# VectorE scales the values' sums one round later, and GpSimd's token operands move one round back

## The reference

```
scores = scale * q @ k.T + bias            # -1e9 outside the window
a = exp(scores - max);  a = a / (sum(a) + 1e-9)
x = a @ v                                  # then tokens x channels
h = x @ w_in;  g = h * sigmoid(h);         x = g @ w_out
h = x @ w_in2; g = h * clip(h + 3, 0, 6) / 6;  out = g @ w_out2
```

## Time and profile before

| | |
|---|---|
| median of 3 runs | 623.41 us (623.38 to 623.52) |
| the profiled execution's own time | 622.65 us |
| its span in the trace | 620.9 us |
| busy: PE, PEld, DVE, ACT, POOL | 94%, 84%, 59%, 54%, 43% |
| TensorE's granted clock | 1.00 of full speed |
| PE busy in the first seven fortieths of the span (0 to 108.7 us) | 80, 70, 70, 60, 70, 70, 60% |
| PE busy in the others | 90% or more, 80% in the last |
| attention on PE | from 5.6 us to about 121 us |

### The profile page before, as it was taken

One profiled execution on the slowest core, in us unless ns is written; L12 is line 12 of the kernel. 1 busy time (PEld: TensorE's weight loads), 2 busy tenths in 40 slices (PEclk: granted clock), 3 DMA queues, 4 the chain that ended last, 5 costly groups with the idle time before them and its releaser, 6 DMA issues.

```text
span 620.9 us, 9690 instructions
## 1 busy us (share of the span) xinstructions
PE 586.5 (94%) x3477; PEld 522.7 (84%) x3477; DVE 365.4 (59%) x680; ACT 335.8 (54%) x661; POOL 266.6 (43%) x279
## 2 busy tenths in 40 slices
PE   8776776999999999999999999999999999999998
PEld 5554555889999999999999998888888888888886
DVE  6455455787665566856755568557555685555431
ACT  5656556754444475644444657555555575445331
POOL 4344454565863333338633334377333333331110
PEclk9999999999999999999999999999999999999999
DMA  8333223013222212221221222222221242221002
GB/s 354 111 138 106 104 103 116 3 40 131 69 82 79 69 43 68 69 78 59 69 75 64 66 69 69 68 70 68 69 69 68 69 150 88 69 68 35 0 1 101
DMA packets 14596, 50.05 MB, mean 81 GB/s; under 512 B 1619, under 2 KB 1875, under 8 KB 14547
## 3 DMA queue, kind: packets, MB, share of 16 engines
q1 hardware_dynamic: 14258, 48.63, 23.1%
q10 hardware_dynamic: 288, 0.79, 0.4%
HBM read 46.27 MB, written 3.15 MB: 80 GB/s over the span
## 4 chain that ended last, share of the span: by engine, by line
PE 87%; ACT 4%; DVE 4%; issue 3%; DMA 1%; ACTq 0%; POOL 0%; DVEq 0%; SPq 0%
PE ps L1038 37%; PE ps L1125 22%; PE ps L1116 13%; PE ps L1117 7%; PE ps L1010 4%; PE ps L986 3%; ACT probs L763 2%; DVE negs L564 1%; ACT probsT L774 1%; PE ps L995 1%; DVE g_lo L694 1%; DMA k_raw<-in_kT 1%; DVE g_f L552 1%; PE ps L976 1%; DVE wi_lo L527 0%
## 5 line engine op out<-in xcount | busy, mean ns | idle before, releaser
L383 POOL TENSOR_TENSOR wo_lo<-wo_raw,wo_hi 128x1024 fp32r<-128x1024 f32 x32 | 77.1, 2410 | 262.4 <-ACT wo_hi L825 255.6
L1038 PE MATMUL ps<-x_hi,wi_hi 128*128 128x384 f32 x448 | 151.2, 337 | 0.7 <-DVE c_sb L542 0.3
L1038 PE MATMUL ps<-x_hi,wi_lo 128*128 128x384 f32 x448 | 150.0, 335 | 0.0
L1038 PE MATMUL ps<-x_lo,wi_hi 128*128 128x384 f32 x448 | 150.0, 335 | 0.0
L542 DVE TENSOR_TENSOR c_sb<-ps,p_c 128x384 f32<-128x384 f32 x64 | 35.7, 557 | 159.8 <-PE ps L1038 159.6
L805 ACT ACTIVATE p_c<-ps 128x384 f32<-128x384 f32 x64 | 31.4, 491 | 128.8 <-PE ps L1038 128.5
L1038 PEld LDWEIGHTS ps<-x_hi,wi_hi 128*128 128x128 f32 x448 | 84.1, 188 | 4.8 <-issue 1.2
L1038 PEld LDWEIGHTS ps<-x_hi,wi_lo 128*128 128x128 f32 x448 | 84.1, 188 | 0.7
L1038 PEld LDWEIGHTS ps<-x_lo,wi_hi 128*128 128x128 f32 x448 | 84.1, 188 | 0.0
L1125 PE MATMUL ps<-wo_hi,g_lo 128*128 128x512 f32 (+1 forms) x194 | 76.3, 393 | 0.0
L1125 PE MATMUL ps<-wo_lo,g_hi 128*128 128x512 f32 (+1 forms) x194 | 76.3, 393 | 0.0
(11 more groups left out here) (104 smaller groups left out, 1108.4 us busy)
## 6 DMA issues: line engine op xcount, KB each, us to landing
wi_raw<-in_w_in SPq DMA_DIRECT2D x32, 512.0 KB, 3.4
wo_raw<-in_w_out SPq DMA_DIRECT2D x32, 512.0 KB, 3.4
v_raw<-in_v SPq DMA_DIRECT2D x8, 704.0 KB, 4.4
k_raw<-in_kT SPq DMA_DIRECT2D x8, 464.0 KB, 5.0
out_y<-y_out SPq DMA_DIRECT2D x11, 256.0 KB, 4.2
q_raw<-in_qT SPq DMA_DIRECT2D x6, 384.0 KB, 5.5
q_raw<-in_qT ACTq DMA_DIRECT2D x2, 384.0 KB, 4.1
out_y<-y_out SPq DMA_DIRECT2D x2, 128.0 KB, 2.0
```

What stands on the lines that cost most here:

```text
L383: nc.gpsimd.tensor_tensor(wo_lo[:, s % 2, :], wo_raw[:, s % 2, :], wo_hi[:, s % 2, :], ALU.subtract).then_inc(wo_lo_ok, 1)
L1038: mm = nc.tensor.matmul(p_bank(bank), w[:, s % 2, at], x[:, b, k, :], start=fresh and k == 0 and i == 0, stop=k == 1 and i == 2, skip_grou ...
```

## The change

It moves work between rounds and adds two waits; no instruction of any engine is added or dropped. VectorE's `x_scaled` moves from four rounds behind to five. GpSimd's token work moves from rounds 15 to 23 into rounds 16 to 23, so that the last round holds three pieces. DVE's low part of B22 also waits for four low parts, and ACT's high part of B22 for four high parts, so that the counting semaphores keep their meaning.

```diff
-X_WORK = {15: (("s", 0, 0), ("s", 0, 1)), 16: (("s", 1, 0), ("h", 0, 0)), 17: (("s", 1, 1), ("h", 1, 0)), 18: (("l", 0, 0),),
...
-          23: (("s", 2, 0), ("s", 2, 1))}
+X_WORK = {16: (("s", 0, 0), ("s", 0, 1)), 17: (("h", 0, 0), ("s", 1, 0)), 18: (("h", 1, 0), ("s", 1, 1)), 19: (("l", 0, 0),),
+          20: (("l", 1, 0),), 21: (("h", 2, 0), ("h", 3, 0)), 22: (("l", 2, 0),), 23: (("l", 3, 0), ("s", 2, 0), ("s", 2, 1))}
...
                 dve.wait_ge(x_hi_ok, 7 * blk + i + 1)
+                if blk == 0 and i == B22:
+                    dve.wait_ge(x_lo_ok, 4)
                 nc.vector.tensor_tensor(x_lo[:, i, :, :], src, x_hi[:, i, :, :], ALU.subtract).then_inc(x_lo_ok, 1)
...
                     u = 2 * r
-                    if r >= 4:
-                        x_scaled(r - 4)
+                    if r >= 5:
+                        x_scaled(r - 5)
...
                         copy_t(2 * r - 3)
+                x_scaled(NR - 5)
                 inverse(NR - 2)
...
+                if blk == 0 and i == B22:
+                    act.wait_ge(x_hi_ok, 4)
                 if i in (T1, T2, T3, T4):
```

More of the change, by code:

```diff
@@ L36 @@
           11: (("h", 1, 0),), 12: (("l", 1, 0),), 13: (("h", 1, 1),), 14: (("l", 1, 1),)}
-X_WORK = {15: (("s", 0, 0), ("s", 0, 1)), 16: (("s", 1, 0), ("h", 0, 0)), 17: (("s", 1, 1), ("h", 1, 0)), 18: (("l", 0, 0),),
-          19: (("l", 1, 0),), 20: (("h", 2, 0), ("h", 3, 0)), 21: (("l", 2, 0),), 22: (("l", 3, 0),),
-          23: (("s", 2, 0), ("s", 2, 1))}
+X_WORK = {16: (("s", 0, 0), ("s", 0, 1)), 17: (("h", 0, 0), ("s", 1, 0)), 18: (("h", 1, 0), ("s", 1, 1)), 19: (("l", 0, 0),),
+          20: (("l", 1, 0),), 21: (("h", 2, 0), ("h", 3, 0)), 22: (("l", 2, 0),), 23: (("l", 3, 0), ("s", 2, 0), ("s", 2, 1))}
 SOON_COPY = {1: 0, 4: 2, 6: 4}
```

## The result

| | before | after |
|---|---|---|
| median, lowest to highest, us | 623.39 (622.61 to 623.52, 4 runs) | 596.15 (595.53 to 596.89, 4 runs) |
| profiled execution: time, span, us | 622.65, 620.9 | 596.89, 595.1 |
| round 5 to the first product, us | 87.96 | 62.91 |
| first product to the next step's | 16.18 | 14.78 |
| from there to the end | 498.96 | 498.93 |

The ratio is 0.9566, with a 95% interval from 0.9549 to 0.9583: the kernel is 4.3% faster. The forecast was 596.4 us.

A forecast was written before the change was run, and what follows sets the result against it. A ring of waits among PE, ACT and DVE was taken to bound attention. Gains 27.4 - 1.9 + 1.5 = 27.0 us from 622.65 gave 595.65, and with 0.76 for the median 596.4 us, give or take 2 (76%); ends 593.7 and 603.

The forecast's parts named there:

- The ring: Attention rounds before: PE, ACT and DVE wait for one another once a round, 4.63 us each; no engine is slow.
- The rounds: Rounds 5 to 23: PE itself becomes the bound, 60.54 us in place of 87.96, a gain of 27.4 us.
- The transfers: Loads of q for rounds 9, 12, 15, 18 and 21 land late and stall PE: 1.9 us back, bounds 0 and 5.3.
- The end of attention: First product to the next step's: PE's wait for ACT's copy goes, 1.5 us gained; bounds 2.3 gained, 0.8 lost.
- The added waits: End of attention: DVE's wait for T1's low part and ACT's wait on POOL's earlier work cost 0.
- A: Attention rounds: copies still hold PE, rounds near 3.53 us, 6.5 us given back, 602.9 us; chance 10%.
- B: Attention pairs: loads bound them, each burst landing at 7.26 us, 3.4 us more, 599.8 us; chance 9%.
- C: Late `x_scaled` holds PE's `turn_inverses`: rounds stay as long, the end gets longer, 626.1 us; chance 2%.
- D: Attention rounds: the change does nothing because PE's values wait for something else at the same moment, 623.4 us; chance 3%.

The follow-up runs named there:

- The last experiment: Kernel before, with ACT's `copy_t(u - 4)` ahead of `exps(u)` from the same round on: 617.94 us, ratio 0.9925.
- the fifth kernel: Kernel after, with `x_scaled(r - 5)` between the second and third pass of the round's four `negated`, not ahead of them: 603.92 us, ratio 0.9689.
- The two experiments on the transfers: Kernel after, k and q loads issued ahead of v: sent as soon as their buffers are free, 593.73 us; in one burst with v last, 594.09 us.
- The first experiment: Kernel before, with only `x_scaled` one round later, GpSimd's table and VectorE's waits as they were: 596.6 us, ratio 0.9575.
- The second: Kernel after with `x_scaled` put back four rounds behind, so only GpSimd's table and the two added waits are new: 623.63 us, ratio 1.0009.

## Why the prediction was right

**The ring.** It was said that no engine is slow, and that `negated` is late because `x_scaled` in front of it waits for the last work of PE's round. The last experiment shortened a link, and the next link held PE. The first only moved the one waiting instruction, and the waits of all three engines shrank together. Both are what a ring does.

**The rounds: 27.4 us forecast, 27.5 without the transfers.** 87.96 - 60.47 in the two kernels that load k and q first. The floor of 60.54 us was a sum of PE's own rows, and it was met to 0.07. The 1.25 us from scores to `negated`, the only estimate in the laying out, is 1.18 (47.69 to 48.87).

**The transfers: 1.9 us forecast, 2.4 measured.** Four stalls of 0.2 us and one of 1.06 were forecast. Over the 3.11-us steps of the kernel without these waits, the rounds 9, 12, 15, 18 and 21 of the kernel after stand 0.17, 0.30, 0.11, 0.28 and 1.45 late, 2.31 together; the round behind each is 0.03 longer (3.36 for 3.33), which makes 2.46. The stalls' number and places were right. Their size owes something to luck: the rows gave 0.12 us, the prediction rounded it up to 0.2, and the mean was 0.22. So does the one late landing among five, which was taken from a single row. The kernel before, the kernel after, the scaling alone and the table alone each show one, but the fifth kernel shows two and the sixth none, so a kernel can have a microsecond more or less of it. Here it came 0.3 us later than the one of the kernel before, as 6.6 and not 6.3 us. The two experiments on the transfers show that this term is theirs alone.

By the Trainium skill, "DMA: Bandwidth & Descriptors", section "Anatomy of one DMA", the term would have been 0. The trace disagrees a second time: q is issued at 55.35, 1.08 us after the round's end at 54.27, and lands 5.3 later, 6.4 us after it and not 5.7. The runs also say in good part where the rule falls short here. From the first issue of the burst, all three (1589 KB in thousands of bytes) take 55.35 + 5.3 - 54.38 = 6.3 us, and k and q alone (868 KB) took 48.41 + 3.9 - 48.04 = 4.3. Two bursts are a weak base: over the on-time bursts of the kernel after and of the two kernels that load k and q first, the times are 6.1 to 6.4 and 4.3 to 4.6 us, 6.23 and 4.37 in the mean. From these means, an estimate: 721 KB more in 1.86 us, some 390 GB/s, and 2.1 us that don't depend on the size. While its DMA engines are fully busy the kernel after moves 369 GB/s (68.10 to 69.10, below). The fixed part is near the 2.0 us of the Trainium skill; the rate is lower than its 436 GB/s, and by this estimate most of the missing half microsecond lies there.

**The end of attention: 1.5 us forecast, 1.40 measured.** The transposes that waited 1.47 us now follow the product at once. PEld's timeline has no bracket there:

```profile
82.37 0.97 PEld L991 LDWEIGHTS ps<-ident,probs 128*128 128x128 f32 x8
```

`total(23)` came 1.31 us after the first product (forecast 1.36). T4's high part, forecast at 9.1, came at 9.5 (90.91): T4's two sums took 2.70 us with a low part of DVE beside them, where the prediction had 2.0 from the kernel before. T4's low part was done at 92.75, and P4 begins at 93.47, so it was in time all the same, with 0.7 us to spare.

**The added waits: 0 forecast.** The first experiment has no added waits and the old table, and it ends attention in the same 14.78 us. The second has them without the lead, and pays 0.7. So the cost is hidden by the lead, as the prediction said for T1's low part, and not nil in itself.

**The rivals.** A, that the copies still hold PE, would leave waits for `probsT` and rounds of 3.53: neither is there. B, the loads at 7.26 all five times, happened once in five. C needs `x_scaled` to come late; the fifth kernel made that so, and the wait appeared where C had put it. D falls with the result.

**Where it was off.** The profiled execution was forecast at 595.65 us and took 596.89. Of the 1.24 us, 0.68 is the late start of round 4, from slower first products of PE, which nothing in the trace of before could tell; 0.5 the transfers; 0.1 the end. The median was nearer, 0.25 off, because this execution was the longest of the four: the medians differ by 27.2 us, the two profiled executions by 25.8. That the forecast of 27.0 met the first so closely is in part luck; the terms themselves are good to about half a microsecond each.

## What to carry to other kernels

When several in-order engines all idle once a period and none is full, look for the instruction that waits for the youngest product of another engine and stands ahead of something that could already run; put it behind work that fills that time, and check what was hidden by the old period. Work out the floor from the bounding engine's own rows: here it held to about 0.1%, and whatever was above it was a transfer that the long rounds had covered. In a burst on one queue, the load that is needed first goes first.

## What the runs showed of the hardware

**One burst in five lands late.** q landed 6.6 us after its issue in the last such burst of the kernel after, against 5.3 to 5.5 in the other four. Windows of one microsecond show how (columns as above; the last two are the DMA engines' busy share and GB/s):

```profile
68.10:69.10 1.00, 1.00 (x11) 0.78 (x8) 0.67 (x3) 0.71 (x5) 0.47 (x3) 1.00 1.01 369
69.10:70.10 1.00, 1.00 (x17) 0.83 (x17) 1.00 (x8) 1.00 (x5) 1.00 (x1) 1.00 0.66 253
70.10:71.10 1.00, 0.34 (x8) 0.09 (x2) 0.81 (x2) 1.00 (x5) 1.00 (x2) 1.00 0.05 18
71.10:72.10 1.00, 0.26 (x2) 0.29 (x4) 0.00 (x0) 0.50 (x3) 0.51 (x3) 1.00 0.04 11
```

The bulk is over by 70.1. Then six packets of the queue (18 GB/s) move in one microsecond and two in the next, while PE stands; most of the 11 GB/s there is one packet of instructions. The granted clock stays at 1.00. Late bursts are in other traces too. Six traces have bursts in the order v, k, q: of their 30, six landed q 6.1 us or more after its issue (6.3 before, 6.6 after, 6.7 with the scaling alone, 6.1 with the table alone, 6.2 and 6.1 in the fifth kernel) and the others at most 5.8. They belong to rounds 15, 18 and 21, so it is not one certain load. Why the last packets of one burst are late stays open; no experiment was aimed at it.

**DVE and GpSimd on the same inputs.** DVE's low part took 0.95 us before, and 1.76 after:

```profile
85.21 1.76 DVE L537 TENSOR_TENSOR x_lo<-x_raw,x_hi 128x768 fp32r<-128x768 f32 x1
```

GpSimd's two sums beside it, from 85.14 on (nanoseconds, shortest, median, longest):

```profile
L374 POOL TENSOR_TENSOR x_t<-x_raw x2: 1021/1376/1732, 85.1 to 86.1; 128x384 f32<-128x384 f32 x2
```

GpSimd started 0.07 us ahead of DVE, and its first sum took its usual 1.02. DVE's instruction ends at 86.97, 0.81 us after that sum's end, so it seems to have begun only there, and GpSimd's second sum then took 1.73. Before, DVE was first (110.96), took 0.95, and only GpSimd's sum beside it was long, 1.70. The Trainium skill, "SBUF — State Buffer", section "Who interferes with whom", says that a DVE instruction with two inputs in SBUF and a GpSimd instruction that reads SBUF exclude each other, the one issued first going through; the trace agrees in both orders. It costs nothing here, with PE as the bound, but it makes a duration read from one order a poor price for the other.
